# Routing of a mixture of experts: positions as one-hot in a low and a high factor

## The chip, the cores and the metric

The kernel runs on one core of a Trainium2 chip. The metric is the device time of one execution in microseconds (us), from the start of the program to its end.

## The reference

Three layers follow each other on 3072 tokens of 512 numbers. The change touches only the assignment of the second. In short:

```
x = attention(q, k, v, mem_k, mem_v)       # 4 x 768 tokens, chunks of 32 with a window; (3072, 512)
logits = x @ w_gate                        # (3072, 8), 8 experts
for idx in argsort(-logits.flatten()):     # greedy, best pairs first, at most 384 tokens per expert
    tok, e = idx // 8, idx % 8
    if assigned[tok] >= 0 or counts[e] >= 384: continue
    assigned[tok] = e; counts[e] += 1
for e in range(8): out[mask_e] = relu(x[mask_e] @ w1[e]) @ w2[e]       # 512 -> 1024 -> 512
h = out @ w_in; solu = h * softmax(h); out = (layernorm(solu) * g_ln) @ w_out
```

## The kernel before

The work has three parts: attention for 24 units of 128 tokens (0 to 131 us), an opening (131 to 174 us) in which the first expert is found and its rows are fetched, and eight experts one after the other. Each expert takes the 384 tokens that were assigned to it, gathered from memory into `gath` as three blocks of 128 rows. Large products are made of three products of float32 parts (high times high, high times low, low times high), written at one helper's lines L574 to L576.

The greedy assignment is done expert by expert. The next expert to fill up is the one whose 384th best logit is highest. For routing f, VectorE and TensorE search that threshold for all experts at once, in 17 rounds (`search`, `count`, `refine`; TensorE adds the counts in `total`, L540). `end_search` and `thresholds` close the search. Then:

- `choose(f)` (VectorE) finds the expert, writes the rows of its weights to be fetched (`w_idx`), and marks in `picked` the tokens above and at the threshold: 128 partitions x 24 columns, twice.
- `ranks(f)` (TensorE) multiplies `picked` by a triangular matrix `before` (L561) and by ones (L562): how many picked tokens stand ahead in the column, and how many are in each column.
- `place(f)` (VectorE) makes positions 0 to 383 of this: a scan over the columns (L1141), sums, -1000 for picked tokens and +1000 later, so that others lie past the capacity; then `third` (position divided by 128) and `pos_b` (the rest), a one-hot `hot_a` of the third times the token's id in two parts (`rhs_id`), and a one-hot `hot_b` of the rest, 24 x 128 elements (L1158). At the end it takes the placed tokens and the filled expert out of the table `M`.
- `token_ids(f)` (TensorE, L568) is 24 products of `hot_b` and `rhs_id`: each token's id lands at its position in the expert, 128 partitions x 6 columns.
- `write_ids(f)` (VectorE) adds the two parts to `ids` (L1181). `best_open(f + 1)` prepares the next table `Vm`, which TensorE transposes in `best_T` (L533); `begin_search` copies it to `VB`.

In a steady expert s the order of each engine is written out by hand. TensorE: 8 h groups, 2 o groups of expert s - 1, 4 y groups, 6 z groups, and the third o group of s - 1. The small products of the routing stand inside the z groups: thresholds after the first step of group 0, ranks inside group 1, token_ids at the end of group 3, best_T after the second step of group 5. `rows_T` (L587) transposes the three gathered blocks in the middle of the last o group. VectorE, at the end of an expert: choose, place, write_ids, best_open, `max_z` 0 and 1, begin_search, one count, `weigh(s, 0)` (L1206, z times its exponential), max_z 2, `row_low` (L1252, the low parts of the rows), and on to the next search rounds; the first h product waits for row_low. GpSimd (`fetch`): two weight fetches (L1382) when `w_idx` is there, three gathers (L1405) when `ids` is there, `weight_lo` (wl, L1388) and fetches in turn, then the scatter of the third block of s - 1 (L1430), which waits for `o_last` from ScalarE, and the other weight parts. Expert 0 has no o group after its z groups.

In the opening TensorE runs ranks, token_ids, best_T, `total(1, 0)`, the transposes of row block 0, `total(1, 1)`, the transposes of blocks 1 and 2, and three products without use (`keep_warm`).

Of the kernel before, what the change touches and what calls it, by code (L numbers as in the profile page):

```python
# [23 lines left out]
F32 = mybir.dt.float32  # L24
# [30 lines left out]
MARK = 1000.0  # L55
WCH = 4
# [43 lines left out]
def build(nc, qk_in, v_in, v_mem, w_gate, w1, w2, w_in, w_out, g_ln, out):  # L100
    ctx = ExitStack()
    with ctx:
# [3 lines left out]
        def sem(name):  # L106
# [11 lines left out]
        iota_p = sb("iota_p", [P, P], BF16)  # L118
        iota_third = sb("iota_third", [P, NT, 6], BF16)
        id_parts = sb("id_parts", [P, NT, 6], BF16)  # L120
# [30 lines left out]
        upto = sb("upto", [P, 2 * NT], F32)  # L151
        pos2 = sb("pos2", [P, 2 * NT], F32)
        pos = sb("pos", [P, NT], F32)
        keep = sb("keep", [P, NT], F32)
        third = sb("third", [P, NT], F32)
        pos_b = sb("pos_b", [P, NT], BF16)
        hot_a = sb("hot_a", [P, NT, 6], F32)
        rhs_id = sb("rhs_id", [P, NT, 6], BF16)
        hot_b = sb("hot_b", [P, NT, P], BF16)
        id_hi = sb("id_hi", [P, TILES], F32)  # L160
# [6 lines left out]
        below = sb("below", [P, 1], I32)  # L167
# [53 lines left out]
        ids_ps = sem("ids_ps")  # L221
        ids_kept = sem("ids_kept")
# [87 lines left out]
                   hot_a[0:G, :, :].rearrange("p t n -> p (t n)").bitcast(BF16)[:, 0:2 * P]]  # L310
        squares = hot_b[:, 0:F // P, :].rearrange("p t n -> p (t n)")
# [17 lines left out]
        cand_16, following_16 = WIDE[:, 400:400 + WAYS].bitcast(I32), WIDE[:, 416:416 + WAYS].bitcast(I32)  # L329
        H_BANK = [g % 3 for g in range(KF)]  # L330
# [109 lines left out]
        def _(pe):  # L440
# [124 lines left out]
            def token_ids(f):  # L565
                pe.wait_ge(hot_ready, f + 1)
                for t in range(NT):
                    mm = nc.tensor.matmul(TOT[:, 16:22], hot_b[:, t, :], rhs_id[:, t, :],  # L568
                                          start=(t == 0), stop=(t == NT - 1))
                mm.then_inc(ids_ps, 1)  # L570

# [102 lines left out]
            def z_group(s, g, routed):  # L674
# [7 lines left out]
                for k in range(KD):  # L682
# [41 lines left out]
            def keep_warm(n):  # L724

                for _ in range(n):
                    nc.tensor.matmul(MM[0][:, :], ones_b[:, :], hot_b[:, 0:4, :].rearrange("p t n -> p (t n)"),
# [209 lines left out]
        def _(ve):  # L937
# [48 lines left out]
            nc.vector.memset(reached[:, :], 16.0)  # L986
            for k, n, turn in ((0, 7, -1), (7, 15, -1 << 31)):
# [116 lines left out]
            def choose(f):  # L1104
# [4 lines left out]
                else:  # L1109
# [4 lines left out]
                                                    op0=ALU.is_equal, op1=ALU.mult))  # L1114
# [392 lines left out]
```

## Time and profile before

| what | value |
|---|---|
| median of 3 runs | 798.73 us (794.93 to 800.34) |
| the profiled execution | 797.4 us, span 795.6 us |
| TensorE busy in the span | 704.5 us (89%) |
| VectorE, ScalarE, GpSimd busy | 558.5, 356.6, 303.0 us |
| `o_last` of successive experts (the chain of waits) | 388.39, 464.22, 540.47, 616.45, 692.40 us: a period of about 75.9 |

Times in rows are microseconds from the start of the span. PE is TensorE's products, PEld its weight loads, DVE is VectorE, ACT ScalarE, POOL GpSimd, SP SyncE. L12 is line 12 of the kernel. A row of the timeline has start, duration, engine, line, operation, output <- inputs, sizes and count; in brackets stands the engine's idle time before it and what released it. Busy time of an engine that nobody waits for costs nothing.

### The profile page before, as it was taken

What the parts mean: (1) busy time and instruction counts of PE and PEld (TensorE: products, weight loads), DVE (VectorE), ACT (ScalarE), POOL (GpSimd) and SP (SyncE); (2) the same over time, 40 slices, a digit from 0 to 9 for tenths busy, and PEclk for the clock granted to TensorE, in tenths of its full rate; (3) what the DMA queues carried; (4) which work ended last, traced back from release to release, by engine and by line L of the source; (5) the groups of instructions that cost most, each with busy time, mean ns of one, the idle gap of its engine ahead of it and who ended that gap; (6) DMA issues with size and microseconds to landing.
All of it is one profiled execution on the core that took longest, in us unless ns stands there. A gap on an engine that the chain in (4) does not pass through costs nothing.

```text
span 795.6 us, 17918 instructions
## 1 busy us (share of the span) xinstructions
PE 704.5 (89%) x7016; PEld 612.3 (77%) x7017; DVE 558.5 (70%) x2061; ACT 356.6 (45%) x567; POOL 303.0 (38%) x221
## 2 busy tenths in 40 slices
PE   3779986359979999899999998999999999999993
PEld 2557664248969888888979897988898989898882
DVE  3458776688688878777887788688869787741150
ACT  2558666424147325622571356136514741563270
POOL 2000001867057207721761375147514740672001
PEclk9999998569999999999999999999999999999997
DMA  8989986142133013301330232033103311330001
GB/s 232 286 252 291 302 251 226 57 145 78 33 104 108 36 53 107 106 28 54 111 102 28 82 106 78 28 93 120 54 29 118 119 54 52 106 108 28 0 14 40
DMA packets 24386, 83.89 MB, mean 105 GB/s; under 512 B 4033, under 2 KB 4097, under 8 KB 24321
## 3 DMA queue, kind: packets, MB, share of 16 engines
q0 software_dynamic: 13056, 46.14, 18.0%
q1 hardware_dynamic: 11264, 36.91, 15.2%
q8 instruction: 37, 0.61, 0.3%
q14 instruction: 29, 0.23, 0.1%
HBM read 70.46 MB, written 12.58 MB: 104 GB/s over the span
## 4 chain that ended last, share of the span: by engine, by line
PE 64%; DVE 11%; POOL 7%; issue 6%; DMA 6%; ACT 3%; SPq 1%; POOLq 0%; DVEq 0%; ACTq 0%
PE bank L574 18%; PE bank L576 16%; PE bank L575 16%; POOL wl L1388 4%; DMA raw<-w,w_idx 4%; PE bank L496 2%; PE banks L478 2%; DMA vr<-v_in 2%; DVE z L1206 2%; PE bank L453 2%; PE bank L463 2%; POOL raw L1382 1%; PE bank L489 1%; PE banks L603 1%; DVE hits L1027 1%
## 5 line engine op out<-in xcount | busy, mean ns | idle before, releaser
L1388 POOL TENSOR_TENSOR wl<-raw,wh 128x1024 fp32r<-128x1024 f32 x60 | 145.1, 2420 | 20.3 <-ACT wh L789 18.9
L1382 POOL DMA_INDIRECT raw<-w,w_idx x60 | 66.2, 1103 | 158.4 <-DVE w_idx L1121 121.4
L574 PE MATMUL bank<-xh,wh 128*128 128x384 f32 x256 | 90.4, 353 | 3.5 <-POOL wl L1388 3.3
L574 PE MATMUL bank<-hh,wh 128*128 128x384 f32 x256 | 90.0, 351 | 0.0
L576 PE MATMUL bank<-xh,wl 128*128 128x384 f32 x256 | 86.7, 339 | 0.0
L575 PE MATMUL bank<-xl,wh 128*128 128x384 f32 x256 | 86.5, 338 | 0.0
L576 PE MATMUL bank<-hh,wl 128*128 128x384 f32 x256 | 85.8, 335 | 0.0
L575 PE MATMUL bank<-hl,wh 128*128 128x384 f32 x256 | 85.8, 335 | 0.0
L789 ACT ACTIVATE wh<-raw 128x1024 fp32r<-128x1024 f32 x60 | 63.3, 1056 | 46.2 <-DMA raw<-w,w_idx 46.0
L574 PE MATMUL bank<-wout_h,uh 128*128 128x512 f32 x192 | 78.7, 410 | 0.2
L574 PE MATMUL bank<-win_h,yh 128*128 128x512 f32 x192 | 77.2, 402 | 0.0
L576 PE MATMUL bank<-wout_h,ul 128*128 128x512 f32 x192 | 75.3, 392 | 0.0
L576 PE MATMUL bank<-win_h,yl 128*128 128x512 f32 x192 | 75.0, 391 | 0.0
L575 PE MATMUL bank<-win_l,yh 128*128 128x512 f32 x192 | 74.9, 390 | 0.0
L575 PE MATMUL bank<-wout_l,uh 128*128 128x512 f32 x192 | 74.8, 389 | 0.0
L883 ACT ACTIVATE yh<-bank 128x384 fp32r<-128x384 f32 x32 | 15.8, 492 | 121.0 <-PE bank L576 121.0
L890 ACT ACTIVATE z<-bank 128x512 f32<-128x512 f32 x48 | 28.7, 598 | 90.3 <-PE bank L576 90.3
L1027 DVE TENSOR_SCALAR_CACHE_REDUCE hits<-VB,bank 96x256 bf16<-96x256 f32 x120 | 57.6, 480 | 4.3
L1368 POOL TENSOR_TENSOR win_l<-prep_first,win_h 128x1024 fp32r<-128x1024 f32 x4 | 9.3, 2342 | 128.6 <-DVE Vm L1078 128.6
L1233 DVE SCALAR_TENSOR_TENSOR hl<-bank,hh 128x384 fp32r<-128x384 f32 x64 | 35.3, 551 | 28.9 <-ACT hh L851 28.9
L574 PEld LDWEIGHTS bank<-xh,wh 128*128 128x128 f32 x256 | 48.8, 191 | 6.3 <-POOL wl L1388 3.5
L1206 DVE SCALAR_TENSOR_TENSOR z<-z,ez 128x1024 f32<-128x1024 f32 x24 | 49.3, 2056 | 3.6 <-ACT ez L805 3.6
(207 smaller groups left out, 1649.4 us busy)
## 6 DMA issues: line engine op xcount, KB each, us to landing
unit<-qk_in SPq DMA_DIRECT2D x24, 768.0 KB, 9.6
vr<-v_in SPq DMA_DIRECT2D x48, 130.0 KB
x_rows<-x_sb SPq DMA_DIRECT2D x24, 256.0 KB, 6.8
prep_first<-w_in SPq DMA_DIRECT2D x4, 512.0 KB, 5.9
vr<-v_mem SPq DMA_DIRECT2D x32, 32.5 KB
prep_first<-w_out SPq DMA_DIRECT2D x2, 512.0 KB, 8.1
prep_rest<-w_out SPq DMA_DIRECT2D x2, 512.0 KB, 9.0
raw<-w,w_idx POOLq DMA_INDIRECT x60, 4.3
```

Of the source, the lines that this page charges most:

```text
L453: mm = nc.tensor.matmul(S_PS[r % 2][a][CHUNK * c:CHUNK * (c + 1), hp * WIN:(hp + 1) * WIN], q[rows, hp, CHUNK * c:CHUNK * (c + 1)], k[rows ...
L463: mm = nc.tensor.transpose(PT_PS[:, hp * P:(hp + 1) * P], pr[:, r % 2, hp, :, :].rearrange("p a w -> p (a w)"), ident[:, :])
L574: nc.tensor.matmul(bank, stat_h, mov_h, start=first, stop=False)
L575: nc.tensor.matmul(bank, stat_h, mov_l, start=False, stop=False)
L576: return nc.tensor.matmul(bank, stat_l, mov_h, start=False, stop=last)
L789: nc.scalar.activation(wh[:, c % WCH, :], stage(s, c), ACT.Copy).then_inc(w_hi, 1)
L890: nc.scalar.activation(z[:, g // 2, 512 * (g % 2):512 * (g % 2) + 512], MM[z_bank(s, g)][:, :], ACT.Copy)\
L1027: ins = nc.vector.tensor_scalar(hits_of[n], VB[:, :], cand[:, n:n + 1].bitcast(F32), None, ALU.is_ge, ALU.add, accum_out=cnt[:, n:n + 1])
L1206: nc.vector.scalar_tensor_tensor(out=z[:, i, :], in0=z[:, i, :], scalar=1.0, in1=ez[:, :], op0=ALU.mult, op1=ALU.mult, accum_out=u_sum[:, ...
L1233: nc.vector.scalar_tensor_tensor(out=hl[:, g, :], in0=MM[H_BANK[g]][:, 0:CAP], scalar=0.0, in1=high(hh[:, g, :]), op0=ALU.max, op1=ALU.sub ...
L1382: gp.indirect_dma_start(stage(s, c), None, table, bass.IndirectOffsetOnAxis(ap=w_idx[:, c % WCH:c % WCH + 1], axis=0))\
L1388: gp.tensor_tensor(wl[:, c % WCH, :], stage(s, c), wh[:, c % WCH, :].bitcast(F32), ALU.subtract)\
```

## The change

The position is split at 32 instead of 128: a low part of 0 to 31 (one-hot of 24 x 32 elements) and a high part of 0 to 11, whose one-hot is multiplied by the two parts of the id (24 x 12 x 2). `token_ids` gives 32 partitions x 24 columns. One more product with a constant `spread` copies these 32 partitions to 4 x 32, and a mask `own_span` with a reduction picks each partition's own value. The marks come from the constants: `before` has -1000 on its diagonal, and the scan begins at +1000. Positions are int32, so that the parts are bit operations. The clean-up of `M` is moved from `place` to `write_ids`. In `choose(0)` `w_idx` is written after `picked`, and the steps to the threshold aren't waited for. In the opening all three row blocks are transposed ahead of `total(1, 1)`.

```diff
+LOW, HIGH = 32, CAP // 32
+SPAN = P // LOW
 def token_ids(f):
     pe.wait_ge(hot_ready, f + 1)
     for t in range(NT):
-        mm = nc.tensor.matmul(TOT[:, 16:22], hot_b[:, t, :], rhs_id[:, t, :], ...)
+        mm = nc.tensor.matmul(TOT[0:LOW, 16:16 + 2 * HIGH], hot_low[:, t, :], rhs_id[:, t, :, :], ...)
     mm.then_inc(ids_ps, 1)
+def spread_ids(f):
+    pe.wait_ge(ids_low_ready, f + 1)
+    nc.tensor.matmul(TOT[:, 48:48 + 2 * HIGH], spread[:, :], id_low[:, :], start=True, stop=True)\
+      .then_inc(spread_ps, 1)
 # z_group
     if routed and (g, k) == (3, 3):
         token_ids(s + 1)
+    if routed and (g, k) == (4, 1):
+        spread_ids(s + 1)
 # tensor, opening
 token_ids(0)
+spread_ids(0)
 best_T(1)
 total(1, 0)
-rows_T(0, [0])
+rows_T(0)
 total(1, 1)
-rows_T(0, [1, 2])
 # choose
+if f == 0:
+    t_max = digit + 15
 done(e_star); e_rows; done(e_hot)
-wait raw_loaded if f > 0; w_idx
-if f == 0:
-    done(digit = digit + 15); done(t_max = digit >> SIXTEEN_SHIFT ^ following_16)
+if f == 0:
+    t_max = t_max >> SIXTEEN_SHIFT ^ following_16
+else:
+    name_weights()                          # the same waits and w_idx
 done(mask); done(val); picked
+if f == 0:
+    name_weights()
 # place
-done(scan(upto, ones48, whole, 0.0)); done(pos2 = upto - whole); done(pos2 += within)
-done(pos2 += picked * -MARK); done(pos = min of the halves)
-done(keep = (pos >= CAP - MARK) * -2 NEG); done(pos += MARK); keep = keep + NEG
-done(third = pos >= 128); done(third += pos >= 256); done(pos_b = pos - 128 * third)
-done(hot_a = iota_third == third)           # 24 x 6
-rhs_id = hot_a * id_parts                   # 24 x 6
-hot_b = iota_p == pos_b                     # 24 x 128, then hot_ready
-done(e_cap); done(M = min(M, e_cap)); done(M = min(M, keep))
+done(scan(upto[1:], ones48, whole, MARK)); done(pos2 = upto[0:48] + within); done(pos = min of the halves)
+pos_low = pos & 31; done(pos_high = pos >> 5)
+done(hot_a = iota_high == pos_high)         # 24 x 12
+rhs_id = hot_a * id_parts                   # 24 x 12 x 2
+hot_low = iota_low == pos_low               # 24 x 32, then hot_ready
+done(keep = (pos >= CAP) * -2 NEG); keep = keep + NEG
 # write_ids, behind the copies of ids_prev
+done(e_cap); done(M = min(M, e_cap))
 ve.wait_ge(ids_ps, f + 1)
-done(id_hi = TOT[:, 19:22]); ids = id_hi + TOT[:, 16:19], then ids_ready
+id_low = TOT[0:32, 16:40], then ids_low_ready
+done(M = min(M, keep))
+ve.wait_ge(spread_ps, f + 1)
+done(id_own = TOT[:, 48:72] * own_span)
+ids = sum(id_own, each of the 3 blocks), then ids_ready
 # GpSimd, start: constants iota_low, iota_high, id_parts (24 x 2), spread, own_span, the diagonal of before
```

Vector instructions are written here as assignments; `done` waits until the instruction has ended.

## Rows read from the trace of the kernel before

**Rows 1.** The table of windows: busy time of each engine, clock, DMA.

```profile
core 0: us, PE busy (x) PEld busy (x) DVE busy (x) ACT busy (x) POOL busy (x), PEclk, DMA share, GB/s
131.00:174.00 43.00, 14.59 (x261) 11.03 (x262) 31.07 (x123) 17.37 (x21) 28.87 (x17) 0.52 0.40 142
...
384.00:460.00 76.00, 74.35 (x422) 66.10 (x421) 61.42 (x239) 33.27 (x53) 35.33 (x24) 1.00 0.24 77
```

**Rows 2.** The timeline of the opening, all engines, 153 to 174 us.

```profile
153.95 0.23 DVE L1121 TENSOR_SCALAR w_idx<-row_base,e_rows 128x4 uint32<-128x4 f32 x1
...
154.45 0.36 DVE L1128 TENSOR_TENSOR mask<-Vm,e_hot 128x192 f32<-128x192 f32 x1
...
155.18 1.13 POOL L1382 DMA_INDIRECT raw<-w,w_idx  x1 [1.30 <-DVE w_idx L1121]
...
156.09 0.25 DVE L1141 TENSOR_TENSOR_SCAN upto<-ones,bank 128x48 f32<-128x48 f32 x1 [0.35 <-PE bank L562]
156.38 0.20 DVE L1142 TENSOR_TENSOR pos<-upto,bank 128x48 f32<-128x48 f32 x1
...
159.11 3.35 DVE L1158 TENSOR_TENSOR hot_b<-iota_p,pos_b 128x3072 bf16<-128x3072 bf16 x1
...
162.52 0.80 PE L568 MATMUL bank<-rhs_id,hot_b 128*128 128x6 bf16 x24 [6.47 <-DVE hot_b L1158]
...
163.62 0.16 DVE L1181 TENSOR_TENSOR ids<-id_hi,bank 128x3 uint32<-128x3 f32 x1
...
170.37 0.24 PE L540 MATMUL bank<-cnt,same_expert 96*96 96x3 bf16 x1 [0.90 <-DVE hot_a L1027]
...
173.92 0.42 PE L574 MATMUL bank<-xh,wh 128*128 128x384 f32 x1 [0.22 <-DVE xl L1252]
```

**Rows 3.** Groups of VectorE by line: busy us, mean ns, idle before.

```profile
L1158 DVE TENSOR_TENSOR hot_b<-iota_p,pos_b 128x3072 bf16<-128x3072 bf16 x8 | 26.8, 3352 | 0.0
...
L1155 DVE TENSOR_TENSOR hot_a<-iota_third,third 128x144 f32<-128x144 bf16 x8 | 2.5, 308 | 0.3
...
L1094 DVE SCALAR_TENSOR_TENSOR bank<-below,hot_b 128x16 int32<-128x16 int32 x1 | 1.7, 1682 | 0.0
```

**Rows 4.** The timeline of a hand-over in the steady part, 374 to 395 us.

```profile
374.83 0.76 PE L568 MATMUL bank<-rhs_id,hot_b 128*128 128x6 bf16 x24
...
375.82 0.16 DVE L1181 TENSOR_TENSOR ids<-id_hi,bank 128x3 uint32<-128x3 f32 x1
...
376.79 0.95 POOL L1405 DMA_INDIRECT gath<-x_rows,ids  x1 [7.70 <-DVE ids L1181]
...
376.93 0.39 PE L574 MATMUL bank<-win_h,yh 128*128 128x512 f32 x1
...
377.12 0.36 DVE L1018 TENSOR_TENSOR Vm<-M,mask 128x192 f32<-128x192 f32 x1
...
379.67 0.38 PE L533 MATMUL bank<-ident,Vm 128*96 128x128 f32 x2
...
380.28 2.40 POOL L1388 TENSOR_TENSOR wl<-raw,wh 128x1024 fp32r<-128x1024 f32 x1
...
380.95 2.82 DVE L1206 SCALAR_TENSOR_TENSOR z<-z,ez 128x1024 f32<-128x1024 f32 x1
...
386.00 1.28 DVE L1252 TENSOR_TENSOR xl<-banks,xh 128x512 fp32r<-128x512 f32 x2
...
388.19 0.33 PE L574 MATMUL bank<-xh,wh 128*128 128x384 f32 x1
...
389.93 1.01 POOL L1430 DMA_INDIRECT out<-o_last,ids_last  x1 [1.12 <-ACT o_last L840]
...
394.42 1.21 DVE L1206 SCALAR_TENSOR_TENSOR z<-z,ez 128x1024 f32<-128x1024 f32 x1
```

**Rows 5.** The timeline of TensorE: rows with an idle time before them.

```profile
235.01 0.41 PE L574 MATMUL bank<-xh,wh 128*128 128x384 f32 x1 [3.25 <-POOL wl L1388]
...
404.57 0.20 PE L540 MATMUL bank<-cnt,same_expert 96*96 96x3 bf16 x1 [1.00 <-DVE hot_a L1027]
```

More of the change, by code:

```diff
@@ L329, in build @@
         cand_16, following_16 = WIDE[:, 400:400 + WAYS].bitcast(I32), WIDE[:, 416:416 + WAYS].bitcast(I32)
+        below = WIDE[:, 440:441].bitcast(I32)
+        hot_low = hot_b[:, :, 0:LOW]
         H_BANK = [g % 3 for g in range(KF)]
@@ L1114, in choose, with name_weights @@
                                                     op0=ALU.is_equal, op1=ALU.mult))
+                def name_weights():
+                    if f > 0:
+                        for i in range(2):
+                            ve.wait_ge(raw_loaded[i], 16 * WCH * f - 32)
+                    nc.vector.tensor_scalar(w_idx[:, :], row_base[:, :], e_rows[:, 0:1], None, ALU.add)\
+                      .then_inc(w_idx_ready, 1)
+                if f == 0:
+                    nc.vector.tensor_scalar(t_max[:, :], digit[:, :], 15.0, None, ALU.add)
                 done(nc.vector.tensor_reduce(e_star[:, :], e_val[:, :], AX.X, ALU.min))
@@ L1140, in place @@
                 ve.wait_ge(ranks_ps, f + 1)
-                done(nc.vector.tensor_tensor_scan(upto[:, :], ones48[:, :], whole, 0.0, ALU.mult, ALU.add))
-                done(nc.vector.tensor_tensor(pos2[:, :], upto[:, :], whole, ALU.subtract))
-                done(nc.vector.tensor_tensor(pos2[:, :], pos2[:, :], within, ALU.add))
-                done(nc.vector.scalar_tensor_tensor(out=pos2[:, :], in0=picked[:, :], scalar=-MARK, in1=pos2[:, :],
-                                                    op0=ALU.mult, op1=ALU.add))
@@ L1178, in write_ids @@
                     nc.vector.tensor_copy(ids_prev[:, :], ids[:, :])
+                done(nc.vector.tensor_scalar(e_cap[:, :], e_hot[:, :], 2.0 * NEG, -NEG, ALU.mult, ALU.add))
+                done(nc.vector.tensor_tensor(M[:, :, :, :], M[:, :, :, :],
+                                             e_cap[:, :].unsqueeze(1).unsqueeze(3).to_broadcast([P, 2, E, TG]), ALU.min))
                 ve.wait_ge(ids_ps, f + 1)
-                done(nc.vector.tensor_copy(id_hi[:, :], TOT[:, 16 + TILES:16 + 2 * TILES]))
-                nc.vector.tensor_tensor(ids[:, :], id_hi[:, :], TOT[:, 16:16 + TILES], ALU.add).then_inc(ids_ready, 1)
+                nc.vector.tensor_copy(id_low[:, :], TOT[0:LOW, 16:16 + 2 * HIGH]).then_inc(ids_low_ready, 1)
+                done(nc.vector.tensor_tensor(M[:, :, :, :], M[:, :, :, :],
+                                             keep[:, :].rearrange("p (j t) -> p j t", j=2).unsqueeze(2)
+                                             .to_broadcast([P, 2, E, TG]), ALU.min))
+                ve.wait_ge(spread_ps, f + 1)
+                done(nc.vector.tensor_tensor(id_own[:, :, :, :].rearrange("p i q b -> p (i q b)"), TOT[:, 48:48 + 2 * HIGH],
+                                             own_span[:, :, :, :].rearrange("p i q b -> p (i q b)"), ALU.mult))
+                with nc.allow_low_precision(reason="the sums are whole numbers below 2**24"):
+                    nc.vector.tensor_reduce(ids[:, :], id_own[:, :, :, :].rearrange("p i q b -> p i (q b)"), AX.X, ALU.add)\
+                      .then_inc(ids_ready, 1)
             first_search()
```

106 lines of the change are left out of this document (56 added, 50 removed).

## The prediction

> **What bounds the kernel now.** I first read the table of windows. From 131 to 174 us, the stretch in which the first search and the first routing run with nothing to hide them, TensorE is busy 14.59 us of 43.00 at clock 0.52; in a middle expert (384 to 460) it is busy 74.35 of 76.00 at clock 1.00 [rows 1]. So there are two regimes. Before 174 us a microsecond taken out of VectorE's chain is a microsecond of the kernel; afterwards TensorE is the bound, and an expert has at most 1.65 us of TensorE idle time in it. The timeline of the opening [rows 2] shows the links of that chain; the timeline around a hand-over in the steady part [rows 4] shows who is how early; the TensorE rows with an idle time [rows 5] show where the engine does wait: 3.25 us once, at the hand-over from expert 0 to 1, and 1.00 us in a middle expert for a count of the threshold search. The reader is to see in rows 4 that TensorE issues the id products at 374.83 with no idle time before them: it is not waiting for the positions.
>
> **The opening, 1: choose.** `choose(0)` loses three waited steps between the winner and the mask (w_idx at 153.95, then +15 and the threshold), 0.5 us up to 154.45, the starting time of the mask three such steps on; two small unwaited steps stay, 0.17. Gain 0.33. The weights' table fetch is moved behind `picked`: w_idx is written about 1.3 us later, and so is issued on GpSimd's queue at about 156.5 instead of 155.18 [rows 2]. Nothing else is queued there until the row gathers, and the weights' low parts are computed only after those; I cost it at nothing. Without that cover it costs 1.3.
>
> **The opening, 2: place.** From the scan at 156.09 to the start of the large one-hot at 159.11 are 3.02 us; the one-hot takes 3.35 [rows 2]. VectorE's price per element is read from two shapes: 3072 elements 3.352 us, 144 elements 0.308 [rows 3], so 1.04 ns an element and 0.16 us of overhead. The new chain: scan to sum 0.29 (156.09 to 156.38), sum 0.24, minimum 0.22, low bits 0.09 (unwaited), high bits 0.22, then 288 elements 0.46 + 0.04 of wait, 576 elements 0.76 - 0.08 of overlap, 768 elements 0.96: together 3.20, against 3.02 + 3.35 = 6.37. Gain 3.17. I take int32 operands at the same price per element; no row has this form. A first use can cost far more: one operation at 136 us took 1.682 us [rows 3], where its like takes 0.2. The new forms may cost 0 to 1.5 us once; I take 0, as most of the forms here show no such excess.
>
> **The opening, 3: ids.** The 24 products (0.80) stay, with 24 moving columns instead of 6. A column costs (0.39 - 0.33)/128 = 0.47 ns at full clock [rows 4], so 24 x 18 columns cost at most 0.2 us, 0.4 at half clock, and perhaps nothing behind the weight loads. Less is possible too: the stationary part has 32 columns, not 128. I take 0. Before, two steps led from the bank to `ids`; now a copy, the product with `spread` (0.24 like the small product at 170.37, about 0.35 until VectorE sees it), a product and a reduction. Ids therefore cost 0.16 + 0.35 + 0.40 instead of 0.36: +0.55. `ids` ends at 163.78 + 0.55 - 0.33 - 3.17 = 160.83, a gain of 2.95. Everything behind it (gather, best_open, first count) moves with it.
>
> **The opening, 4: order.** TensorE waits for a count at 170.37 before it transposes row blocks 1 and 2 (idle 0.90 [rows 2]). With all blocks first, block 1 starts at its landing and the last VectorE part of the rows is up to 0.7 earlier. The count is not due yet, so nothing waits for it. VectorE's own search then sets part of the pace, and the clock rises only around 174; so of 2.95 + 0.7 I take 3.3, with 1.5 (a slow first use, a late clock) to 3.8 as ends.
>
> **The steady part, 1: where `ids` goes.** The hand-over looks as if 2.4 us of VectorE were saved there too. They are not worth anything by themselves, since the id products are issued at their place behind z group 3 in any case: 374.83 to 375.59 [rows 4]. What matters comes after. Before, `ids` was complete at 375.82 + 0.16 = 375.98. Now `spread` stands in TensorE's program behind the second step of z group 4; the products of the third step start at 376.93 [rows 4], so `spread` runs there. VectorE sees it at about 377.15 and needs two steps, 0.4: `ids` at 377.55. That is **1.57 us later** than before (bounds 1.3, if the bank is seen at once, and 1.8). TensorE is 1.34 us behind the id products by its own order alone, and waits for nothing. The queue behind the wait on VectorE is best_open, two row maxima, begin_search, the count and `weigh`; on GpSimd the gathers, w-low 0, two weight fetches, w-low 1 and the scatter.
>
> **The steady part, 2: what the delay meets.** `Vm` was ready at 377.12 + 0.36 = 377.48; 1.57 later is 379.05, before TensorE transposes it at 379.67: hidden. GpSimd's w-low 0 moves from 380.28 to 381.85. `weigh` moves from 380.95 by some 1.25 (a wait of 0.3 was there) to 382.2. `weigh` took 2.82 us where it began behind w-low 0 and 1.21 us alone at 394.42 [rows 4]: its end is tied to the end of w-low, 2.40 + 1.1 us after its start. The Trainium skill (SBUF — State Buffer, Who interferes with whom) says that a VectorE instruction with two inputs in SBUF and a GpSimd instruction that reads SBUF exclude each other for the whole instruction and that issue order decides who blocks; these two rows agree. So the whole 1.57 passes through to the last part of the rows' low halves, less 0.3 of wait: from 386.00 + 1.28 = 387.28 to 388.58. The h products began at 388.19 [rows 4] with no wait; they now begin at about 388.75. TensorE loses 0.5.
>
> **The steady part, 3: the scatter.** GpSimd stood idle 1.12 us before the scatter at 389.93 [rows 4], which waits for o_last and so for TensorE. The queue ahead of it is now 1.57 later, less that idle time and with the 0.3 us issue spacing: the scatter starts about 0.8 later, and w-low 2 and 3, the fetches and the high parts behind them with it. That chain ends in the count for which TensorE waited 1.00 us at 404.57 [rows 5]. The two losses are parallel, so the later one counts: 0.8 for each of experts 2 to 7, with `spread` itself (0 to 0.2, taken as 0.1) included: **+4.8**; bounds 0 and 6 x 1.57 = 9.4.
>
> **The steady part, 4: expert 0 to 1.** There is no o group to cover the hand-over: the 3.25 us before 235.01 [rows 5] are waited for the same chain (the page names w-low 1; the last low part of the rows ends within 0.15 us of it). All of 1.57 shows: **+1.6**, bounds 1.3 and 2.6, since more idle time can keep the clock at its 1.2 GHz level longer.
>
> **Sum.** -3.3 + 1.6 + 4.8 = +3.1 us. On the profiled execution, 797.4 us with a span of 795.6, that is 800.5. It lies 1.3 under the median of the three runs, 798.73, to which the difference is applied: 801.8. One per cent is 8 us, about what a measurement of this kernel can tell from no change.
>
> **The rivals.**
> - A, the delay is absorbed (22 in 100). For it: `Vm` has 0.6 us of slack, the scatter 1.12, the rows 0.9. Against it: each is below 1.57. Then only the opening (-3.3) and expert 0 to 1 (+1.6), or not even this, remain: 798.7 - 1.7 = 797.0, at best 795.
> - B, the change of order between `weigh` and w-low 0 (10 in 100). The margin was 0.67 us (380.28 to 380.95) and is 0.35 by my sum. If `weigh` comes first, it is done in 1.21, but w-low 0 starts about 1.5 us later still, the scatter chain with it: +2.3 for each of six experts instead of 0.8, 13.8 - 1.7 = +12: 811. It decides from 0.35 us of shift between the two. The rule of the Trainium skill named above (SBUF — State Buffer, Who interferes with whom) describes the same mechanism.
> - C, the whole 1.57 shows in each hand-over (12 in 100): -3.3 + 1.6 + 9.4 = +7.7: 806.4.
> - D, `ids` is not later, because TensorE or VectorE stands otherwise than I read, and VectorE's saved time is given back in full as in the usual reading of such a change: 2.4 us in each hand-over can at most remove the waits for counts, 1.65 an expert: -3.3 - 10 = 785.5 (6 in 100). Against it: at the id products TensorE does not wait.
>
> **How the numbers follow.** The main case has 50 in 100 (801.8, itself 798 to 805). A reaches down to 795, C up to 807. The range 794 to 807.5 leaves out B, D and some of the tails. Faster by over 1% (below 790.7): D and little else, 0.07. Slower by over 1% (above 806.7): B and half of C, 0.15. Within 1%: 0.78.
>
> **What the changed profile would show.** The first h product about 3.3 us earlier, near 170.6. One-hot of 768 elements near 0.96 us. In a middle expert: id products at the same distance behind z group 3; `ids` 1.9 us behind them instead of 0.4; the gather 1.6 us later against the z products; `weigh` still behind w-low 0 with some 2.8 us; an idle row of TensorE at the first h product, about 0.5; the period from one hand-over to the next near 76.7 instead of 75.9. Wrong would make me: `ids` not later, or later without an idle row; a clock that stays low after the opening; a slow first use.

## The result and the profile after

The changed kernel takes 802.16 us, the median of 20 runs (798.23 to 806.91), the kernel before 798.77 us (20 runs, 794.93 to 803.93). The ratio is 1.0044, with a 95% interval of 1.0026 to 1.0062: 3.5 us slower, between 2.1 and 5.0. The forecast was 801.8, the change 3.1 us slower. Its profiled execution took 804.62 us with a span of 802.9, which is 2.5 us above its own median; that of before was 1.4 below its. So the two traces differ by more (7.3 us of span) than the kernels do, and the reading below has to say which part of the 7.3 belongs to the change.

The table of windows of the changed kernel stands beside [rows 1]:

```profile
131.00:174.00 43.00, 18.46 (x278) 14.16 (x279) 29.85 (x128) 17.37 (x21) 30.83 (x18) 0.52 0.44 158
171.00:174.00 3.00, 2.80 (x9) 2.67 (x9) 1.99 (x12) 0.00 (x0) 2.84 (x2) 0.50 0.84 292
190.00:200.00 10.00, 8.31 (x40) 7.61 (x39) 7.09 (x37) 1.93 (x3) 4.41 (x2) 0.83 0.00 0
236.00:242.00 6.00, 4.97 (x16) 4.87 (x17) 4.21 (x22) 1.59 (x3) 4.33 (x3) 0.50 0.46 154
384.00:460.00 76.00, 74.26 (x418) 65.26 (x417) 58.16 (x236) 32.55 (x54) 34.48 (x23) 1.00 0.23 75
```

VectorE is busy 58.16 us of a middle expert instead of 61.42, 3.3 less; the large one-hot alone accounts for 2.4 of it (0.97 instead of 3.35). TensorE, which is the bound, is busy as before. The rows from 171, 190 and 236 us show what the opening's gain ran into, and the same windows of the kernel before are these:

```profile
171.00:174.00 3.00, 2.56 (x10) 1.56 (x10) 1.58 (x5) 1.19 (x2) 2.67 (x3) 0.51 0.50 164
190.00:200.00 10.00, 8.26 (x49) 7.68 (x48) 8.35 (x45) 3.01 (x5) 4.70 (x2) 1.00 0.00 0
236.00:242.00 6.00, 6.00 (x29) 5.83 (x29) 4.13 (x24) 3.26 (x6) 4.06 (x3) 0.77 0.28 89
```

The opening of the changed kernel, beside [rows 2] (timeline, VectorE and TensorE):

```profile
152.28 2.19 DVE L1145 TENSOR_SCALAR e_hot<-iota_e,e_star 128x8 f32<-128x8 f32 x1
...
156.21 0.26 DVE L1167 TENSOR_TENSOR_SCAN upto<-ones,bank 128x48 f32<-128x48 f32 x1 [0.22 <-PE bank L570]
...
158.49 0.97 DVE L1177 TENSOR_TENSOR hot_b<-iota_low,pos_low 128x768 bf16<-128x768 int32 x1
...
159.51 0.81 PE L576 MATMUL bank<-rhs_id,hot_b 128*32 128x24 bf16 x24 [3.34 <-DVE hot_b L1177]
160.66 0.19 PE L584 MATMUL bank<-id_low,spread 32*128 32x24 bf16 x1 [0.33 <-DVE id_low L1198]
...
161.18 0.18 DVE L1206 TENSOR_REDUCE ids<-id_own 128x3 uint32<-128x24 f32 x1
...
171.36 0.66 PE L589 MATMUL bank<-xh,wh 128*128 128x384 f32 x1 [0.20 <-DVE xl L1278]
```

The scan is still at 156, the one-hot of 768 elements takes 0.97 us instead of 3.35, and the first h product comes at 171.36 instead of 173.92. The start of the routing moves a little from one execution to the next (the copy into `M`, from which the opening runs, is at 132.05 before and 132.61 here), so I measure from that copy: `ids` ends 31.73 us behind it before and 28.75 after, a gain of 2.98, and the first h product 41.87 and 38.75, a gain of 3.12. But that product now takes 0.66 us, where before it took 0.42: it is issued at the 1.2 GHz level, which lasts up to 174 in this profile.

The hand-over in the steady part, beside [rows 4] (timeline, all engines):

```profile
377.07 0.39 PE L591 MATMUL bank<-win_h,yl 128*128 128x512 f32 x1
377.38 0.76 PE L576 MATMUL bank<-rhs_id,hot_b 128*32 128x24 bf16 x24
378.08 0.50 PE L589 MATMUL bank<-win_h,yh 128*128 128x512 f32 x1
378.41 0.40 PE L590 MATMUL bank<-win_l,yh 128*128 128x512 f32 x1
...
379.34 0.40 PE L591 MATMUL bank<-win_h,yl 128*128 128x512 f32 x1
379.67 0.18 PE L584 MATMUL bank<-id_low,spread 32*128 32x24 bf16 x1
379.78 0.50 PE L589 MATMUL bank<-win_h,yh 128*128 128x512 f32 x1
380.12 0.40 PE L590 MATMUL bank<-win_l,yh 128*128 128x512 f32 x1
...
380.18 0.18 DVE L1206 TENSOR_REDUCE ids<-id_own 128x3 uint32<-128x24 f32 x1
...
381.17 0.96 POOL L1443 DMA_INDIRECT gath<-x_rows,ids  x1 [9.62 <-DVE ids L1206]
...
384.66 2.41 POOL L1426 TENSOR_TENSOR wl<-raw,wh 128x1024 fp32r<-128x1024 f32 x1
...
384.94 3.22 DVE L1232 SCALAR_TENSOR_TENSOR z<-z,ez 128x1024 f32<-128x1024 f32 x1
...
390.00 1.28 DVE L1278 TENSOR_TENSOR xl<-banks,xh 128x512 fp32r<-128x512 f32 x2
...
391.39 0.19 PEld L589 LDWEIGHTS bank<-xh,wh 128*128 128x128 f32 x1 [0.46 <-issue]
...
393.50 1.02 POOL L1468 DMA_INDIRECT out<-o_last,ids_last  x1 [0.30 <-issue]
...
408.02 0.20 PE L548 MATMUL bank<-cnt,same_expert 96*96 96x3 bf16 x1 [1.05 <-DVE hot_a L1045]
```

From the id products to the gather it is 381.17 - 377.38 = 3.79 us instead of 1.96 [rows 4]. `weigh` is still behind w-low 0 and takes 3.22. The low parts of the rows end at 391.28, and the first weights of the h products are loaded right after, at 391.39. The scatter at 393.50 starts 16.12 us behind the id products, 15.10 before [rows 4]: 1.02 later, forecast 0.8. But the wait for the count at 408.02, to which the forecast had tied it, is 1.05 us, as good as the 1.00 before [rows 5]. What I had not expected stands at the top: the starts of the large products on either side of the small ones are further apart than usual. Large products follow each other at 0.23 us; from 379.34 to 380.12, a stretch of two such distances, which need 0.45, are 0.78 us. The next section shows what that is.

`o_last` starts at 314.25, 391.39, 468.23, 545.09, 622.16 and 699.35: a mean period of 77.02. By the same rule that of before is 76.18, from 311.52 over the five values of the table of before. (Those five values alone give 76.0; the 75.9 beside them is a little low.) The hand-over from expert 0 to 1, beside [rows 5] (timeline of TensorE, rows with an idle time):

```profile
231.83 0.66 PE L602 MATMUL banks<-ident,gath 128*128 128x128 f32 x4 [0.40 <-DMA gath<-x_rows,ids]
...
237.03 0.66 PE L589 MATMUL bank<-xh,wh 128*128 128x384 f32 x1 [3.61 <-POOL wl L1426]
```

Cut at the same five events, the two spans differ as follows (each column is a difference of starts read from the timelines; h0 and h1 are the first h products of experts 0 and 1, o1 and o6 the first and last `o_last` of the six listed):

| us | start to M | M to h0 | h0 to h1 | h1 to o1 | o1 to o6 | o6 to end | span |
|---|---|---|---|---|---|---|---|
| before | 132.05 | 41.87 | 61.09 | 76.51 | 380.88 | 103.20 | 795.6 |
| after | 132.61 | 38.75 | 65.67 | 77.22 | 385.10 | 103.55 | 802.9 |
| difference | +0.56 | -3.12 | +4.58 | +0.71 | +4.22 | +0.35 | +7.3 |

"h0 to h1" holds chance. Two things of the clock vary in it. The first is where the clock rises after the opening. I read it from windows of 1 us: in the eight profiles that have the changed opening and no added products without use (the changed kernel and kernels 2, 3, 5, 6, 8, 9 and 10 below) the low level lasts from 0.0 to 3.8 us into the h products, 1.9 in the mean; in the two with the old opening (before and kernel 1) 0.0 and 1.1 us. The second is a fall later on. In the profiles of 12 kernels of this case the granted clock from 190 to 200 us, behind a wait of TensorE of about 1.7 us, is 1.00 in six and 0.83 in six, whatever the version (before had 1.00, the changed kernel 0.83). A mean of 0.83 over 10 us is 3.4 us at half speed, about 1.7 us of work lost. The first column is taken as chance too: it runs from 129.94 to 137.08 in these profiles, and the large values aren't tied to a version.

### The profile page after: what moved, and what is told of

The parts are those of the page before. It is cut to its first block, busy times and chain, and to the rows that moved or that the text cites. A ratio compares the mean times of both kernels' runs of the same rounds, so it can differ in the third digit from the quotient of the medians.

```text
span 802.9 us, 17934 instructions
## 1 busy us (share of the span) xinstructions
PE 715.4 (89%) x7025; PEld 615.9 (77%) x7025; DVE 538.4 (67%) x2038; ACT 358.2 (45%) x567; POOL 303.8 (38%) x230
## 4 chain that ended last, share of the span: by engine, by line
PE 62%; DVE 9%; POOL 8%; DMA 8%; issue 7%; ACT 3%; SPq 1%; POOLq 0%; DVEq 0%; ACTq 0%
PE bank L589 17%; PE bank L591 16%; PE bank L590 16%; POOL wl L1426 5%; DMA raw<-w,w_idx 5%; PE bank L504 2%; POOL raw L1420 2%; PE banks L486 2%; DMA unit<-qk_in 2%; PE bank L461 2%; DVE z L1232 2%; PE bank L471 1%; DMA vr<-v_in 1%; PE bank L497 1%; PE banks L618 1%
```

## The experiments

Ten kernels ran, in three sessions beside their own runs of the kernel before (797.59, 798.13 and 797.32 us, 23 to 30 runs each). All ratios are to those; the changed kernel itself was not run again beside them, so a variant is set against it by its trace or by its ratio to before.

**1. The kernel before with later id products.** All of the old arithmetic, but `token_ids` at the place where the changed kernel has `spread`. It isolates the place from everything else.

```diff
-    if routed and (g, k) == (3, 3):
+    if routed and (g, k) == (4, 1):
         token_ids(s + 1)
```

> The kernel before, with nothing changed but the place of the id products on TensorE: behind the second step of z group 4 instead of behind z group 3, so that the ids are ready about 1.37 us later in every hand-over. The opening is as before. Theory (the lateness of the ids is what costs in the steady part, through the row low parts and the scatter): hand-over 0 to 1 +1.4, each of six others +0.55, together +4.7 us on before (3.5 to 6.5), first scatter chain later by 0.5. Rival (the delay is absorbed by the slack, and the changed kernel is slower for another reason: its operations, its longer PE work): 0 to +1.4 us.

Measured: 801.59 us, ratio 1.0050 [1.0026, 1.0075]: 4.0 us. The timeline of its hand-over:

```profile
379.78 0.76 PE L568 MATMUL bank<-rhs_id,hot_b 128*128 128x6 bf16 x24
...
381.74 0.95 POOL L1405 DMA_INDIRECT gath<-x_rows,ids  x1 [9.06 <-DVE ids L1181]
...
385.51 3.22 DVE L1206 SCALAR_TENSOR_TENSOR z<-z,ez 128x1024 f32<-128x1024 f32 x1
...
391.96 0.19 PEld L574 LDWEIGHTS bank<-xh,wh 128*128 128x128 f32 x1 [0.44 <-issue]
```

The same picture as in the changed kernel (`weigh` 3.22, the weights of the h products loaded after 0.44 us of idling), though not one vector instruction is new. Later ids alone, without the opening's gain, cost about what the whole change costs. In the steady part they cost less, though: the mean period is 76.42, 0.24 more than before, where the theory had 0.55 for each hand-over and the changed kernel has 0.84.

**2. The changed kernel with earlier id products.**

```diff
-    if routed and (g, k) == (3, 3):
+    if routed and (g, k) == (2, 3):
         token_ids(s + 1)
-    if routed and (g, k) == (4, 1):
+    if routed and (g, k) == (3, 1):
         spread_ids(s + 1)
```

> The changed kernel, with the id products one z group earlier (behind group 2) and the spread product behind the second step of group 3: ids 2.75 us earlier than in the changed kernel, 0.9 earlier than before. Theory (lateness costs): the period falls from 77.0 to 75.9 to 76.1, hand-over 0 to 1 gets at least what it lost back, and the opening's gain of about 2 us is left: 796.5 us, 2 to 3 us below before. Rival (new operations or longer PE work cost 1 us in each expert): period stays near 77, 802 us.

Measured: 795.82 us, ratio 0.9956 [0.9931, 0.998]. The sign of the change turns with the place of two small pieces of TensorE's program. The mean period falls to 76.34, not to the 75.9 to 76.1 of the theory: the z groups keep the length that the change gave them (18.26, table below). The timeline of its hand-over, VectorE and GpSimd:

```profile
378.50 0.96 POOL L1443 DMA_INDIRECT gath<-x_rows,ids  x1 [6.90 <-DVE ids L1206]
...
382.00 2.41 POOL L1426 TENSOR_TENSOR wl<-raw,wh 128x1024 fp32r<-128x1024 f32 x1
...
383.12 0.41 DVE L1041 COPY VB<-bank 96x256 f32<-96x256 f32 x1 [1.68 <-issue]
383.99 1.52 DVE L1232 SCALAR_TENSOR_TENSOR z<-z,ez 128x1024 f32<-128x1024 f32 x1
...
388.44 0.69 DVE L1278 TENSOR_TENSOR xl<-bank,xh 128x512 fp32r<-128x512 f32 x1 [1.61 <-ACT xh L815]
```

The gather starts 4.19 us ahead of TensorE's transposes of `Vm` (382.69), in the changed kernel 1.46 (382.63), before 2.88 [rows 4]. The last rows show the room by their waits: VectorE now stands idle 1.68 before it copies those transposes (the row names no releaser; the copy starts 0.43 behind their start) and 1.61 for ScalarE. `weigh` begins 0.42 us before w-low 0 ends (382.00 + 2.41) and takes 1.52, not 3.22. In all three kernels it ends 1.09 to 1.10 us behind the end of w-low 0: 383.77 and 382.68 before [rows 4], 388.16 and 387.07 in the changed kernel, 385.51 and 384.41 here.

**3. The changed kernel with the scatter later in GpSimd's queue.** The third block's scatter stands behind w-low 2 and the fetch after it.

```diff
                 for c in range(2, 2 * WCH):
                     weight_lo(s, c)
                     if not first and c + 2 < 2 * WCH:
                         fetch_weights(s, c + 2)
+                    if c == 2 and s >= 2:
+                        scatter(s - 2, 2, ids_last[:, :])
 ...
-                if not first:
-                    scatter(s - 1, 2, ids_prev[:, 2:3] if last else ids_last[:, :])
+                if last:
+                    scatter(s - 1, 2, ids_prev[:, 2:3])
```

> The changed kernel, with the scatter of the third block moved on GpSimd's queue behind weight part 2 and fetch 4 of the next expert, so that these no longer wait for o_last behind it. Theory (the scatter chain sets the count for which TensorE waits 1 us in the h groups): weight part 2 starts about 1.0 us earlier, the idle rows of 1.05 us go or shrink, the period falls by 0.6 to 1.0: 796 to 799 us. Rival (the row low parts and VectorE's own rounds set it): less than 0.2 a period, 801 us or more.

Measured: 803.97 us, ratio 1.0075 [1.005, 1.0101]; the mean period is 76.81, only 0.2 less (the kernels with the same order of the steady part, 4, 5 and 8, have 76.95, 76.89 and 76.98, so even this is hardly clear of chance). The wait of 1.05 us for a count (at 408.02 in the changed kernel) is gone, but another took its place:

```profile
409.05 0.66 PE L618 MATMUL bank<-ident,z 128*128 128x128 f32 x4 [0.66 <-DVE ul L1271]
```

So the 0.8 us that I had hung on the scatter chain came from elsewhere.

**4. Products without use in the opening.** Seven of them behind `spread_ids(0)`, to raise the clock before the first h product.

```diff
             spread_ids(0)
+            keep_warm(7)
             best_T(1)
```

> The changed kernel, with seven more products without use (512 columns) in the opening, between the spread product and the transposes of the table, where TensorE stood idle for 3.2 us. Theory (in the changed kernel the first 2.6 us of h products ran at the 1.2 GHz level, since TensorE was busy too little before them): the clock is 1.00 when they start, 1.3 us less than the changed kernel: 800.9 us, span of the first h groups shorter by 1.3. Rival (the rise has nothing to do with the products put there, or another drop of the clock takes its place): 802.2 us.

Measured: 804.44 us (7 runs), ratio 1.0074 [1.0045, 1.0103]: no gain. From 160 to 171 us the clock is 0.66 instead of 0.50, from 171 to 176 it is 0.62, and the first h product takes 0.66 us, the duration of the low level: the clock rose at about 164.6 and had fallen again at 168, before it was needed.

**5. The spread product issued twice.** To find what the wider pitch around it is.

```diff
+                nc.tensor.matmul(TOT[:, 48:48 + 2 * HIGH], spread[:, :], id_low[:, :], start=True, stop=True)
                 nc.tensor.matmul(TOT[:, 48:48 + 2 * HIGH], spread[:, :], id_low[:, :], start=True, stop=True)\
                   .then_inc(spread_ps, 1)
```

> The changed kernel with the spread product issued twice in a row (the same result, nothing left out). It measures what one such product costs TensorE inside the z groups, which grew from 17.72 us to 18.25 by the change. Theory (a product with 32 rows of stationary part between full ones costs some 0.33 us): z stage 18.4 to 18.6, period +0.1 to +0.35 on the changed kernel. Rival (the growth comes from the id products with 24 columns, and a spread product costs 0.1 like a count): 18.35 or less.

Measured: 803.34 us, ratio 1.0075 [1.0048, 1.0102]. The timeline of TensorE:

```profile
377.84 0.40 PE L592 MATMUL bank<-win_h,yl 128*128 128x512 f32 x1
378.17 0.18 PE L584 MATMUL bank<-id_low,spread 32*128 32x24 bf16 x1
378.21 0.17 PE L585 MATMUL bank<-id_low,spread 32*128 32x24 bf16 x1
378.31 0.50 PE L590 MATMUL bank<-win_h,yh 128*128 128x512 f32 x1
378.65 0.40 PE L591 MATMUL bank<-win_l,yh 128*128 128x512 f32 x1
```

The second product starts 0.04 us behind the first, and the two full products are 0.81 apart instead of 0.78. The z groups take 18.27 us instead of 18.25, so the theory as written (18.4 to 18.6) missed; the result lies in the rival's range, though not for the rival's reason, as kernel 9 shows. A second product of the same shape adds 0.03; the 0.33 of the first are paid once.

**6 and 7. A full stationary part for the spread product, with early ids.** `spread` and `id_low` get 128 rows, with zeros below the 32. The second kernel adds products without use all through the opening (7, 2, 2 and 2).

```diff
-spread = sb("spread", [LOW, P], BF16)
+spread = sb("spread", [P, P], BF16)
-id_low = sb("id_low", [LOW, 2 * HIGH], BF16)
+id_low = sb("id_low", [P, 2 * HIGH], BF16)
+nc.vector.memset(id_low[:, :], 0.0)                  # once
-nc.vector.tensor_copy(id_low[:, :], TOT[0:LOW, ...)
+nc.vector.tensor_copy(id_low[0:LOW, :], TOT[0:LOW, ...)
 # the second kernel
             spread_ids(0)
+            keep_warm(7)
             best_T(1)
+            keep_warm(2)
             total(1, 0)
-            rows_T(0)
+            rows_T(0, [0]); keep_warm(2); rows_T(0, [1]); keep_warm(2); rows_T(0, [2])
             total(1, 1)
```

> The kernel with early ids (id products behind z group 2, spread behind the second step of group 3), and the spread product with all 128 rows of the stationary part, the 96 others zero. Theory (it is the part of the array, 32 rows, that makes the gap of 0.1 us ahead of it): z stage 18.25 falls by 0.1, and the total is 0.5 to 0.8 us under the kernel with early ids, 3.5 to 4.5 under before. Rival (any small product costs this): z stage stays at 18.25.

> The same, and in the opening products without use at each place where TensorE stood idle after the spread product (7, 2, 2, 2 and the old 3), since with 7 alone the clock rose and fell again before the h products. Theory (continuous work keeps the level): first h products at 2.4 GHz, 1.3 us less than without; 5 under before. Rival (the clock falls again, or the added products delay the transposes by as much): no gain.

Measured: 795.89 us, 0.9972 [0.9952, 0.9993], and 794.92 us, 0.9963 [0.9935, 0.9992]. The z groups take 18.07 us in both, 0.18 less than 18.25, where the theory had 0.1. The totals fall short of the expectations (2.2 and 3.0 us under before by the ratios, where 3.5 to 4.5 and 5 had been expected), and kernel 6 is not below kernel 2 in its ratio (0.9972 and 0.9956, with intervals that overlap): what the padding of `spread` saves shows in the traces, not in the total. In the second the clock is 1.00 from 171 to 174 us and the first h product takes 0.41. The gain of 1.0 us between the two lies inside the intervals; in the profile of the first the clock had by chance risen early as well (1.00 from 171 to 176), so the traces can't decide it either.

**8. The old order of the row transposes in the opening.**

```diff
             total(1, 0)
-            rows_T(0)
+            rows_T(0, [0])
             total(1, 1)
+            rows_T(0, [1, 2])
```

> The changed kernel with the old order in the opening (row block 0, count, row blocks 1 and 2). Theory (the new order gives 0.7 us): from the last id step to the first h product 0.7 us more than the changed kernel's 10.0, total +0.7 and not clear of noise. Rival (rows land later than the count anyway): 0.

Measured: 804.34 us (6 runs), ratio 1.0078 [1.005, 1.0106]. M to h0 is 38.79 us, against 38.75 in the changed kernel. The new order is worth 0.04.

**9 and 10. A full stationary part for the id products too,** with the ids at the change's place (9) and early (10). The stationary part takes 128 columns from `hot_b`; what stands behind the 32 of the one-hot only gives sums that nobody reads.

```diff
-mm = nc.tensor.matmul(TOT[0:LOW, 16:16 + 2 * HIGH], hot_low[:, t, :], ...)
+mm = nc.tensor.matmul(TOT[:, 16:16 + 2 * HIGH], hot_b[:, t:t + 2, :], ...)     # 2 x 64 columns
 # hot_b one tile longer and cleared once; `steps` gets a place of its own; spread and id_low as in 6
```

> The changed kernel with both of its new products given a full stationary part: the 24 id products take 128 columns (32 of the one-hot, the rest leftovers whose results nobody reads) instead of 32, and the spread product takes 128 rows (zeros below the 32) instead of 32. Places unchanged. Theory: TensorE pays about 0.1 us each time it goes from products with the full 128x128 stationary part to one with fewer rows or columns, and again on the way back. Then the z groups take 17.85 to 17.95 us instead of 18.25 (17.72 before; 18.07 with the spread product alone full), and 6 x 0.35 = 2 us of the time go: near 800. Rival: the id products cost more for their 24 moving columns, so that only the 0.18 of the spread product comes back: 18.07, and some 801. The waits at the hand-over stay as in the changed kernel in both.

> The same two full stationary parts with the id products one z group earlier and the spread product one group earlier, at the second step of group 3. Theory: z groups 17.9 us instead of 18.07, and about 1 us less than the early version with the spread product alone full: 794 to 795.5, ratio to before 0.995 to 0.997. Rival (moving columns): 18.07 and no difference from that version.

Measured: 799.42 us, 1.0029 [1.0003, 1.0054], and 792.18 us, **0.9940 [0.9916, 0.9963]**. The timeline of TensorE in kernel 9:

```profile
373.13 0.39 PE L591 MATMUL bank<-win_h,yl 128*128 128x512 f32 x1
373.36 0.77 PE L576 MATMUL bank<-rhs_id,hot_b 128*128 128x24 bf16 x24
373.98 0.47 PE L589 MATMUL bank<-win_h,yh 128*128 128x512 f32 x1
374.29 0.39 PE L590 MATMUL bank<-win_l,yh 128*128 128x512 f32 x1
...
375.19 0.39 PE L591 MATMUL bank<-win_h,yl 128*128 128x512 f32 x1
375.42 0.19 PE L584 MATMUL bank<-id_low,spread 128*128 128x24 bf16 x1
375.46 0.47 PE L589 MATMUL bank<-win_h,yh 128*128 128x512 f32 x1
375.78 0.39 PE L590 MATMUL bank<-win_l,yh 128*128 128x512 f32 x1
```

Around the spread product it is 0.59 us from 375.19 to 375.78 (0.78 with 32 rows), around the id products 1.16 from 373.13 to 374.29 (1.34 with 32 columns, from 377.07 to 378.41 in the changed kernel, and 1.17 in the kernel before, from 374.60 to 375.77, whose stationary part was full and whose moving part had 6 columns). These distances are the same at every hand-over of every profile of this case, wherever no record is missing: 0.77 to 0.78 around `spread` with 32 rows (0.80 to 0.81 where it is issued twice) and 0.58 to 0.59 with 128, 1.34 to 1.35 around the id products with 32 columns and 1.15 to 1.17 with 128. The 18 additional moving columns cost nothing. The z groups take 17.85 us. Kernel 9 came out as its theory had it; kernel 10, expected at 794 to 795.5, is faster than that. It has the changed kernel's arithmetic and is 4.8 us faster than the kernel before, and it is the fastest here. Most of that is the place of the ids: between kernels 2 and 10, which differ in the padding, the ratios (0.9956 and 0.9940) have intervals that overlap.

The stages of a middle expert (the second period; each number is the distance between the first products of two stages), three of the six parts of the span, how long the low clock lasts from h0 on, and the clock from 190 to 200:

| | z groups | third o | h groups | M to h0 | h0 to h1 | o1 to o6 | low clock from h0 | clock 190 to 200 |
|---|---|---|---|---|---|---|---|---|
| before | 17.72 | 6.92 | 20.26 | 41.87 | 61.09 | 380.88 | 0.0 | 1.00 |
| after | 18.25 | 7.17 | 20.48 | 38.75 | 65.67 | 385.10 | 2.7 | 0.83 |
| 1 before, ids later | 17.72 | 7.13 | 20.48 | 41.87 | 64.43 | 382.09 | 1.1 | 0.83 |
| 2 ids earlier | 18.26 | 6.93 | 20.38 | 38.75 | 61.79 | 381.69 | 3.5 | 1.00 |
| 3 scatter later | 18.25 | 7.17 | 20.33 | 38.76 | 63.31 | 384.07 | 0.0 | 1.00 |
| 4 products without use | 18.25 | 7.17 | 20.40 | 38.90 | 64.48 | 384.77 | 3.6 | 1.00 |
| 5 spread twice | 18.27 | 7.17 | 20.52 | 38.76 | 64.63 | 384.43 | 3.8 | 1.00 |
| 6 spread full, ids earlier | 18.07 | 6.93 | 20.33 | 38.71 | 62.30 | 380.73 | 1.0 | 0.83 |
| 7 the same, products without use | 18.07 | 6.93 | 20.21 | 38.53 | 60.87 | 381.73 | 0.0 | 1.00 |
| 8 old order of transposes | 18.25 | 7.18 | 20.51 | 38.79 | 65.27 | 384.89 | 1.9 | 0.83 |
| 9 full, ids as changed | 17.85 | 7.28 | 20.46 | 38.89 | 64.35 | 383.42 | 1.0 | 0.83 |
| 10 full, ids earlier | 17.84 | 6.93 | 20.45 | 38.71 | 62.03 | 378.87 | 1.7 | 0.83 |

The z groups and the third o group are the same in all periods of a profile, within 0.02 us. The h groups aren't: in the five periods before they take from 20.24 to 21.31 us.

## Why the prediction was right, point by point

**The opening: right in its steps.** `ids` was forecast 2.95 us earlier and came 2.98 earlier; the one-hots take 0.46, 0.76 and 0.97 as priced, int32 operands at the same price. The first h product was forecast 3.3 earlier and came 3.12 earlier, since the order of the transposes, for which 0.35 had been taken, gives 0.04 (kernel 8). The weights' fetch behind `picked` cost nothing seen here: it is issued at 156.99 instead of 155.18, and the queue stood idle for 3.10 us ahead of the first gather at 162.52. The first use also stayed out of the sum, for a reason that I hadn't given: the step at L1112 (L1094 before) takes 0.18 instead of the 1.68 of [rows 3], and `e_hot`, 0.76 before, takes 2.19. The excess moved; together they are 2.37 and 2.44. (The changed kernel also keeps `below`, an input of that step, in a bank instead of a tile of its own; whether this moved the excess is not shown.)

**What the opening's gain was worth: less.** I named a late clock as a bound and took none. In this pair of profiles the clock rises at 174 in both, so 2.6 us of h products, 171.36 to 174, run at the 1.2 GHz level: about 1.3 us of the 3.1 are handed back. That is one draw. By the column "low clock from h0" the mean is 1.9 us of low clock with the changed opening (0.0 to 3.8) and 0.6 with the old one (0.0 and 1.1), so that some 0.7 us are handed back in the mean, an estimate from eight and two profiles. The added products without use did raise the clock early: it rises between 164 and 165 in kernels 4 and 7, and not before 169 in the ten profiles without them. In kernel 7, where they were spread over the whole stretch, it stayed up to the first h product (0.41), in kernel 4, where they stood in one place, it fell again (0.66). Each is one profile, and neither total shows a gain.

**Where `ids` goes in the steady part: right, and the core of it.** Forecast: 1.57 later, behind TensorE's own order. Measured: 3.79 - 1.96 = 1.83. Of the 0.26 between them, 0.19 are TensorE's way back from the id products and into `spread` (`spread` starts 379.67 - 377.38 = 2.29 behind them, forecast 2.10; with both padded, in kernel 9, it is 2.06), the rest VectorE's sight of the bank (379.96 - 379.67 = 0.29, forecast 0.22). The place decides the sign: kernel 1 has the place without the change and loses 4.0 us; 9 and 10 differ in the place alone, and in 7.2 us (799.42 and 792.18). That Vm's delay is hidden, that `weigh` stays behind w-low 0 and that the low parts of the rows set the h products were as forecast. `weigh` takes 1.21 alone, 2.82 where it starts 0.67 behind w-low 0, 3.22 where it starts 0.28 behind it, 1.52 where it starts 2.0 behind it; its end is 1.07 to 1.10 us behind that of the w-low in all 12 profiles, wherever it starts 0.25 to 2.0 us behind the start of one that takes its usual 2.4. The blocking goes the other way too: before, the `weigh` at 242.78 takes its 1.21, and the w-low that starts at 242.77 takes 3.48 instead of 2.40. The traces so agree with the rule quoted in the prediction from the Trainium skill (SBUF — State Buffer, Who interferes with whom).

**The size of a hand-over: right by luck in part.** 0.8 for each of six, 4.8 in all. The five whole periods give 4.22, 0.84 each; with h1 to o1 (+0.71) it is 4.93, but that column holds clock as well, as the point on expert 0 to 1 says. The terms are others than mine. In the middle expert of the table, TensorE's z groups grow by 0.53 (I had 0.1 for `spread` and nothing for the id products), the wait for the rows' low parts costs 0.25 (I had 0.5) and the h groups grow by 0.22. The first two are the same in every period. The third is not: over five periods the h groups grow by 0.15 in the mean, and in kernel 1 by 0.02, so it isn't clear of chance. Kernel 1, with the old products, has the wait (0.21) and not the longer z groups. The step that failed is **the scatter**: "the two losses are parallel, so the later one counts: 0.8" rested on the chain behind the scatter. The scatter did start 1.02 later, but the count at its end was waited for 1.05 us instead of 1.00, and kernel 3, which takes the scatter out of that chain, gains about 0.2 or less. What held 0.8 up was the term that I had set at "0 to 0.2, taken as 0.1". Kernels 5, 6, 9 and 10 show what it is: going from a full 128 x 128 stationary part to one with 32 rows and back costs 0.19 us (0.78 - 0.59), to one with 32 columns 0.18 (1.34 - 1.16), once for each stay, not for each product. By the z groups it is 0.18 (18.25 to 18.07) and 0.22 (18.07 to 17.85); the 0.13 that are left of 0.53 are the spread product itself with a full part (0.59 - 0.45 = 0.14). I read the price of a small product in the opening, where TensorE waits on both sides of it and such a switch can't show.

The Trainium skill (TensorEngine Tiling (Array Packing), Tiling Modes, Key Properties) states that a change of the tiling mode drains TensorE, though it gives no time for it. The traces fit this: `spread` with 32 rows starts 0.33 behind the large product ahead of it, with 128 rows 0.23, and the second large product behind it comes 0.45 and 0.36 later, so 0.10 us going in and 0.09 coming back. No row records a mode, so that this is the reason is a reading; the cost and what removes it are measured. A rule that looks nearer would have misled: by the Trainium skill (TensorE: Matmul & The Clock Gate, Why this matters for your kernels) a single product with a contraction of 32 takes the same time as one of 128. The durations here do agree (0.18 and 0.19 us); the pitch of the neighbours doesn't. The changed kernel's count products, 96 rows by 96 columns, don't pay: from 386.07 to 386.64 are 0.57 us, no more than around a padded `spread` (0.59). The timeline:

```profile
386.07 0.39 PE L591 MATMUL bank<-wout_h,ul 128*128 128x512 f32 x1
386.30 0.17 PE L548 MATMUL bank<-cnt,same_expert 96*96 96x1 bf16 x1
386.33 0.48 PE L589 MATMUL bank<-wout_h,uh 128*128 128x512 f32 x1
386.64 0.40 PE L590 MATMUL bank<-wout_l,uh 128*128 128x512 f32 x1
```

**Expert 0 to 1: right, but for the clock.** Forecast +1.6, measured +4.58 in the one pair of profiles. Of this 1.3 are the late clock above and 1.7 the fall of the clock between 190 and 200, which the change doesn't cause as far as six against six profiles tell. That leaves 1.6. The same estimate for the others (h0 to h1, less half of the low clock from h0, less 1.7 where the clock fell, against before) gives 1.5 to 2.2 for the four kernels with the changed order of the steady part (3, 4, 5 and 8), 1.1 for kernels 1 and 9, and -0.2 to -1.6 for the four with early ids (2, 6, 7 and 10). The bound of 2.6, "since more idle time can keep the clock at its 1.2 GHz level longer", was needed, one column on: in the changed kernel the clock falls at 235.5, ahead of the first h product at 237.03, and is low up to 242.3; before it falls at 235.4, just behind that product at 235.01, and is low up to 238.8. That is 5.3 us of low clock under h products instead of 3.4, about 0.9 us of work, and it lies in the column h1 to o1 (+0.71). In five of the 12 profiles the clock fell ahead of the first h product, and TensorE had waited 3.31 to 3.61 us for it; in the other seven it fell behind it, after waits of 2.94 to 3.38.

**The rivals.** A (absorbed, 797.0) is out by the interval. B (the order of `weigh` and w-low 0 turned) didn't happen: 384.66 and 384.94, a margin of 0.28 where I had 0.35. C (the whole delay shows, 806.4) fell: 0.25 of 1.83 shows, and at most 0.22 more. D (VectorE's saving is given back, 785.5) fell for the change as it stands; of its number, kernel 10 finds 4.8 us and not 13, with the ids early.

Forecast sum: -3.3 + 1.6 + 4.8 = +3.1. Measured by the same terms in this pair of profiles, and without the fall of 1.7: -3.1 + 1.3 (clock) + about 1.6 + 4.9 = +4.7, with the column behind o6 (+0.35) about 5. The forecast had the clock at nothing; without its 1.3 and the 0.9 inside 4.9 the same sum would be +2.5. In the mean of the profiles the first of the two is 0.7. The 20 runs say 3.5 [2.1, 5.0]. The four variants of the changed kernel that should hardly differ from it (3, 4, 5 and 8) have ratios of 1.0074 to 1.0078, some 6 us, in other sessions. Whether the true difference is nearer to 3.5 or to 5 stays open; the forecast is inside the interval, below its middle.

## What to carry over

A faster producer is worth nothing where its consumer is issued at a written place in another engine's program: move that place with it (here 7.2 us). Before splitting such a step in two, look at which written place the second half will have to stand, and what starts behind it. Give a small product among large ones the full 128 x 128 stationary part, with zeros or leftovers in it, if its neighbours have it (here 0.40 us of each expert's z groups, too little to show in the total). When a stage in front of the bound is shortened, ask at which clock the bound will run in the time that it wins.

## What the runs showed of the hardware

- Leaving the full stationary part and coming back costs TensorE 0.19 us with 32 rows and 0.18 with 32 columns, at full clock and at every hand-over of the profiles; staying there for a second product 0.03; a stationary part of 96 x 96 shows no such cost (0.57 against 0.59 us).
- 24 moving columns instead of 6 cost nothing in a product with 128 stationary columns (1.16 against 1.17 us for 24 of them with their neighbours).
- A `weigh` on VectorE (128 x 1024, both inputs in SBUF) that starts 0.25 to 2.0 us into a w-low of GpSimd ends 1.07 to 1.10 us behind it, and so takes 3.2 to 1.5 us instead of 1.21. Started together with a w-low it took 1.21, and the w-low 3.48 instead of 2.40.
- An excess of about 1.5 us on the first execution of a VectorE step of 0.2 us stands on another step when the program changes (L1094 in before and kernel 1, `e_hot` in the ten others); the sum of the two is 2.33 to 2.45 us in all of them.
- After one and the same wait of 1.7 us (1.69 to 1.77), TensorE's clock fell to its lower level for 3.4 us in six profiles and not in six others: 1.7 us of difference between runs of like kernels.
